# Regrouping seven products and twelve output triples in the second MLP of an attention-MLP kernel

## What is computed

```python
h = x @ w_in;  x = (h - tanh(h)) @ w_out                         # first MLP
h = x @ w_in;  sp = log1p(exp(h))                                # second MLP (sp = h above 20)
out = (h * tanh(sp)) @ w_out
```

## Time and profile before

| | us |
|---|---|
| median of 3 runs | 827.98 |
| lowest, highest | 826.56, 829.07 |
| profiled execution | 828.11 |
| its span | 826.3 |
| TensorE matmuls busy in it | 809.6 |
| VectorE busy | 544.3 |
| ScalarE busy | 363.7 |
| GpSimd busy | 149.8 |

### The profile page before, as it was taken

How to read it: one execution, slowest core, us unless ns; L and a number is a source line. 1 busy time by engine, 2 the same in 40 slices (tenths; PEclk the granted TensorE clock), 3 DMA queues, 4 the chain that set the end, 5 groups by cost and what they waited for, 6 DMA issues and landing times.

```text
span 826.3 us, 13419 instructions
## 1 busy us (share of the span) xinstructions
PE 809.6 (98%) x5340; PEld 761.8 (92%) x5340; DVE 544.3 (66%) x821; ACT 363.7 (44%) x571; POOL 149.8 (18%) x212
## 2 busy tenths in 40 slices
PE   4999999999999999999999999999999999999998
PEld 3999999999999999999999888888988888988896
DVE  5766555555556555534446788888877777877775
ACT  4544434433343434334335455546435445535434
POOL 3230344424404423410110021110000000000000
PEclk9999999999999999999999999999999999999999
DMA  7553345425434534422655255488424266523302
GB/s 249 169 173 112 103 160 202 164 101 192 167 115 167 179 119 160 180 65 90 230 175 182 90 194 202 151 326 309 180 90 159 109 253 240 207 90 120 148 1 77
DMA packets 41597, 132.21 MB, mean 160 GB/s; under 512 B 7104, under 2 KB 10944, under 8 KB 41536
## 3 DMA queue, kind: packets, MB, share of 16 engines
q1 hardware_dynamic: 29088, 83.38, 28.3%
q0 software_dynamic: 12448, 47.98, 16.5%
HBM read 91.49 MB, written 35.91 MB: 154 GB/s over the span
## 4 chain that ended last, share of the span: by engine, by line
PE 89%; DVE 6%; ACT 2%; DMA 1%; issue 1%; SPq 1%; DVEq 0%; ACTq 0%
PE psum L909 8%; PE psum L911 8%; PE psum L910 8%; PE psum L896 7%; PE psum L898 7%; PE psum L897 7%; PE psum L1030 7%; PE psum L1031 7%; PE psum L1029 7%; PE psum L1008 6%; PE psum L1009 6%; PE psum L1007 6%; PE psum L863 1%; PE psum L832 1%; DMA pool_words<-kT 1%
## 5 line engine op out<-in xcount | busy, mean ns | idle before, releaser
L651 DVE TENSOR_TENSOR pool_words<-psum,pool_words 128x384 f32<-128x384 f32 x96 | 53.4, 557 | 121.7 <-ACT pool_words L457 121.7
L909 PE MATMUL psum<-g_hi,w_hi 128*128 128x384 f32 x384 | 128.4, 334 | 0.6 <-DMA pool_words<-pool_words 0.6
L911 PE MATMUL psum<-g_hi,w_lo 128*128 128x384 f32 x384 | 128.3, 334 | 0.0
L910 PE MATMUL psum<-g_lo,w_hi 128*128 128x384 f32 x384 | 128.3, 334 | 0.0
L896 PE MATMUL psum<-x_hi,w_hi 128*128 128x384 f32 x360 | 122.2, 339 | 0.7 <-DVE w_lo L598 0.7
L897 PE MATMUL psum<-x_lo,w_hi 128*128 128x384 f32 x360 | 120.3, 334 | 0.0
L898 PE MATMUL psum<-x_hi,w_lo 128*128 128x384 f32 x360 | 120.3, 334 | 0.0
L457 ACT ACTIVATE pool_words<-psum 128x384 f32<-128x384 f32 x96 | 46.9, 489 | 147.8 <-PE psum L898 144.8
L1008 PE MATMUL psum<-w_lo,w_hi 128*128 128x384 f32 x288 | 97.5, 339 | 0.0
L1009 PE MATMUL psum<-w_hi,w_lo 128*128 128x384 f32 x288 | 97.0, 337 | 0.0
L1007 PE MATMUL psum<-w_hi 128*128 128x384 f32 x288 | 96.3, 334 | 0.0
(11 more groups left out here) (105 smaller groups left out, 1525.4 us busy)
## 6 DMA issues: line engine op xcount, KB each, us to landing
w_hi<-s_hi SPq DMA_DIRECT2D x24, 896.0 KB, 4.6
w_lo<-s_lo SPq DMA_DIRECT2D x24, 896.0 KB, 6.8
pool_words<-w_out POOLq DMA_DIRECT2D x32, 256.0 KB, 3.9
w_hi<-t_hi SPq DMA_DIRECT2D x18, 384.0 KB, 5.0
w_lo<-t_lo SPq DMA_DIRECT2D x18, 384.0 KB, 5.8
pool_words<-w POOLq DMA_DIRECT2D x24, 256.0 KB, 3.7
pool_words<-qT SPq DMA_DIRECT2D x18, 256.0 KB, 3.6
pool_words<-kT SPq DMA_DIRECT2D x18, 256.0 KB, 4.4
```

The costliest lines, as they stand in the source:

```text
L909: pe.matmul(ps, w_hi[:, 1, cols], g_hi[:, s, :], start=f == 0, stop=False)
L910: pe.matmul(ps, w_hi[:, 1, cols], g_lo[:, s, :], start=False, stop=False)
L911: mm = pe.matmul(ps, w_lo[:, 1, cols], g_hi[:, s, :], start=False, stop=f == FT - 1)
```

## The change

TRIPLES_AFTER goes from (2, 2, 1, 1, 1, 3, 2) to (0, 4, 0, 4, 0, 4, 0). With the order M1, M6, M7, M4, M2, M5, M3 this gives, in pairs 2 to 23: M1 M6, four triples, M7 M4, four triples, M2 M5, four triples, M3, and at once M1 and M6 of the next pair. Twelve triples a pair, as before; none follows M3. The order in pairs 0 and 1 on TensorE stays, and the waits of all products and triples are the same in number and place.

The loops of ScalarE and VectorE are written anew for iterations 2 to 24, and iterations 0 and 1 are written out ahead of them. Iteration `pair` now begins with the square term of the upper unit and take_c12 of the pair before. The diff:

```diff
@@ -40,7 +40,7 @@
 
 TOKEN_STEPS = (M1, M5, M3, M7, M6, M2, M4)
 
-TRIPLES_AFTER = (2, 2, 1, 1, 1, 3, 2)
+TRIPLES_AFTER = (0, 4, 0, 4, 0, 4, 0)
 
 
 FIRST_SCORES_AT = 1
@@ -561,32 +561,38 @@
                 act.activation(out_sb[:, j, :], y2_ps[j], ACT.Copy).then_inc(out_kept_act, 1)
 
             act.preload_act_table_set("natural_log_exp_and_others")
-            for pair in range(ALL_PAIRS + 1):
+            keep_m1(0)
+            u_exp(0)
+            inverse(0)
+            u_exp(1)
+            unit_hi(0)
+            inverse(1)
+            keep_y(GROUPS - 1)
+            keep_m1(1)
+            unit_hi(1)
+            u_exp(2)
+            for pair in range(2, ALL_PAIRS + 1):
+                upper, lower = 2 * pair - 2, 2 * pair - 1
                 seam = pair // PAIRS - 1 if pair % PAIRS == 1 and pair > PAIRS else None
-                if pair > 0:
-                    u_exp(2 * pair - 1)
-                if 1 < pair < ALL_PAIRS or pair == 0:
+                inverse(upper)
+                if pair < ALL_PAIRS:
                     keep_m1(pair)
+                u_exp(lower)
+                unit_hi(upper)
                 if seam is not None:
                     keep_out(seam, 0)
-                if pair > 0:
-                    unit_hi(2 * pair - 2)
-                    inverse(2 * pair - 1)
-                if pair == 1:
-                    keep_y(GROUPS - 1)
-                    keep_m1(pair)
+                inverse(lower)
                 if seam is not None:
                     keep_out(seam, 2)
+                unit_hi(lower)
+                if seam is not None:
                     keep_out(seam, 4)
-                if pair > 0:
-                    unit_hi(2 * pair - 1)
                 if pair in LATE_STEP_AT:
                     step_hi(LATE_STEP_AT[pair])
                 if pair in LATE_SPLIT_AT:
                     split_w2_out_hi(LATE_SPLIT_AT[pair])
                 if pair < ALL_PAIRS:
                     u_exp(2 * pair)
-                    inverse(2 * pair)
             for j in range(0, OUT_TILES, 2):
                 keep_out(SUPERS - 1, j)
 
@@ -771,46 +777,55 @@
                     dve.wait_ge(out_stored[j], 16 * s)
                 dve.tensor_copy(out_sb[:, j, :], y2_ps[j]).then_inc(out_kept_dve, 1)
 
-            for pair in range(ALL_PAIRS + 1):
+            for take in (take_u2, take_u3, take_c21, take_c11, take_c22):
+                take(0)
+            clamp(0)
+            square_term(0)
+            take_c12(0)
+            clamp(1)
+            gate(0)
+            square_term(1)
+            unit_lo(0)
+            keep_y(GROUPS - 1)
+            gate(1)
+            take_u2(1)
+            take_u3(1)
+            take_c21(1)
+            unit_lo(1)
+            take_c11(1)
+            take_c22(1)
+            clamp(2)
+            for pair in range(2, ALL_PAIRS + 1):
+
+                upper, lower = 2 * pair - 2, 2 * pair - 1
                 seam = pair // PAIRS - 1 if pair % PAIRS == 1 and pair > PAIRS else None
-                if pair > 0:
-                    gate(2 * pair - 2)
-                    square_term(2 * pair - 1)
-                if 1 < pair < ALL_PAIRS or pair == 0:
+                square_term(upper)
+                take_c12(pair - 1)
+                clamp(lower)
+                gate(upper)
+                if pair < ALL_PAIRS:
                     take_u2(pair)
+                square_term(lower)
+                unit_lo(upper)
                 if seam is not None:
                     keep_out(seam, 1)
-                if pair > 0:
-                    unit_lo(2 * pair - 2)
-                if 1 < pair < ALL_PAIRS or pair == 0:
+                if pair < ALL_PAIRS:
                     take_u3(pair)
-                if pair == 1:
-                    keep_y(GROUPS - 1)
-                if pair > 0:
-                    gate(2 * pair - 1)
-                if pair == 1:
-                    take_u2(pair)
-                    take_u3(pair)
+                    take_c21(pair)
                 if seam is not None:
                     keep_out(seam, 3)
-                if pair < ALL_PAIRS:
-                    take_c21(pair)
-                if pair > 0:
-                    unit_lo(2 * pair - 1)
+                gate(lower)
+                unit_lo(lower)
                 if seam is not None:
                     keep_out(seam, 5)
-                if pair < ALL_PAIRS:
-                    take_c11(pair)
                 if pair in LATE_STEP_AT:
                     step_lo(LATE_STEP_AT[pair])
                 if pair in LATE_SPLIT_AT:
                     split_w2_out_lo(LATE_SPLIT_AT[pair])
                 if pair < ALL_PAIRS:
+                    take_c11(pair)
                     take_c22(pair)
                     clamp(2 * pair)
-                    square_term(2 * pair)
-                    take_c12(pair)
-                    clamp(2 * pair + 1)
             for j in range(1, OUT_TILES, 2):
                 keep_out(SUPERS - 1, j)
 
```

## The result

Over 22 runs each, the changed kernel takes 829.76 us (median; 827.66 to 830.88) and the kernel before 827.07 us. The ratio is 1.003 with a 95% interval of 1.0023 to 1.0037, so the change costs 1.9 to 3.1 us. The forecast was 829.6 us.

A forecast was written before the change was run, and what follows sets the result against it. The prediction took TensorE, busy 809.6 of 826.3 us, as the bound. Matmul density -2.65, new waits +3.25, seam copies +0.15 and the end +0.85 sum to +1.6 us on 827.98: forecast 829.6 us, range 827.0 to 832.3.

The forecast's parts named there:

- density: TensorE, 22 pairs: fewer changes between 384- and 512-column matmuls save 0.12 us a pair, -2.65 us in all.
- waits of pairs 3 to 8: M6 waits for take_c12 behind VectorE's token steps and splits: 4.05 us, less 0.78 of present waits, +3.25 us.
- seams: Two pairs behind a seam: three copies join the queue, two of them behind take_c21, +0.15 us for both.
- end: After pair 23's last M3, only twelve triples cover the chain to unit 47: +0.85 us, from +0.7 to +1.4.
- the product behind four triples: TensorE: the product following a run of four triples pays extra, between 0 and 0.03 us, taken as 0.015.
- The ring: Cycle from one take_c12 to the next through TensorE and VectorE: 15.95 us in iterations 3 and 6, against TensorE's 15.61.
- The 0.60 for the sum: Iterations 2, 4 and 5: GpSimd's token add makes the clamp end 0.60 us later, raising the stall to 0.94.
- M3's waits: Product M3 waiting for take_c22 in pairs 2 to 8 of the kernel before: 0.78 us, which would go.
- Rival A: M6 misses take_c12 in every pair, by 0.15 us in 15 pairs: +2.25, 831.9 us; chance 0.15.
- Rival B: The matmul density gain does not come, because change of width is not the cost: 832.2 us; chance 0.08.
- rival C: VectorE's queue is looser than added up, pairs 3 to 8 stall no more than now: 826.4 us; chance 0.12.
- D: The change only trades one wait for another and pairs keep 15.73 us: 828.0 us; chance 0.05.

The follow-up runs named there:

- runs-of-two kernels: Kernel before with tuple (2, 2, 2, 0, 2, 2, 2): alone 827.08 us; with step_lo and split behind clamp(upper) and old tuple in pair 23, 825.0 us.
- The short sums: Changed kernel with the third super's GpSimd token sums over 8 columns instead of 384; one run, M1(2) to M1(9) 111.08 us.
- the early step_lo: Changed kernel with step_lo ahead of take_u3, the split behind clamp(upper) and step_hi moved forward on ScalarE; 825.6 us, ratio 0.9977 to the kernel before.
- the first experiment: Changed kernel with step_lo and the split moved behind clamp(upper) on VectorE; 830.41 us, ratio 1.0034 to the kernel before.
- the grouping alone: Kernel before with only TRIPLES_AFTER changed to (0, 4, 0, 4, 0, 4, 0), old VectorE and ScalarE queues; 829.15 us, ratio 1.0017.

## Why the prediction was right

Each term of the forecast that has bounds lies within them.

| term | forecast | measured |
|---|---|---|
| density, 22 pairs | -2.65 (-3.5 to -1.2) | -1.91 |
| waits of pairs 3 to 8, less those of before | +3.25 | +3.2 |
| seams | +0.15 | +0.12 |
| end | +0.85 | +0.75 |
| sum | +1.6 | +2.2 |

- **Density.** The step that was mis-sized is the product behind four triples, "I take 0.015, the middle". It pays about 0.026, near the upper bound of 0.03, as behind three triples: 3 x 0.067 us in a pair instead of 3 x 0.055. That makes 22 x 0.087 us. The idea that fewer changes of width bring the gain was incomplete: the runs-of-two kernels have twice as many runs and the same pace. By the starts in the timelines, less the dense pace, a run with the product behind it costs 0.040 us for one triple, 0.033 for two, 0.066 for three and 0.067 for four. What makes a run of two so cheap was not looked into.
- **The ring.** Forecast 0.34 for iterations 3 and 6, 0.94 for 2, 4 and 5 and 0.55 for 7; measured 0.33, 0.93 and 0.55. The short sums show the same ring without GpSimd, and the early step_lo takes both parts away. The 0.60 for the sum was right in size because its rows had the order that the changed kernel has: the split ahead of the sum, the clamp behind it. The reading that a split "that starts inside the add is not blocked" was wrong; the first experiment failed on it. The ring as summed is that of the new queues: with the old ones, in "the grouping alone", the same total falls on other pairs.
- **M3's waits** are gone from pairs 3, 5 and 6, as forecast.
- **The end.** M1(23) to the last triple is 0.66 us longer, and without pair 23's own density gain of 0.09 it is the 0.75 of the table. The waits are 1.01 us ahead of unit 46 and 0.39 ahead of unit 47, each with 0.1 for the slow second matmul. The chain from M3 is 0.6 us shorter, where 0.5 was taken.
- **Rival A** did not happen, but by 0.05 us, less than the 0.1 that the forecast put. Rival B is ruled out by the quiet pairs and rival C by pairs 3 to 8. D's exchange of one wait for another is real, yet the quiet pairs are faster.
- **The base.** The forecast counted from 827.98, the median of the three runs shown; over 22 runs it is 827.07. So its +1.6 us stands against a measured +2.5 (1.9 to 3.1) and lies below the interval, by the density term above all (0.74 us). That 829.6 is so near the measured 829.76 is luck: a base 0.9 us too high and a change 0.9 us too small cancel. The traces show +2.2, so some 0.3 us of the runs' difference has no place in the sum.

## What to carry to other kernels

Where the bound engine's stream is dense, add up the ring through the queue that feeds it before regrouping. Here a product that reuses a bank one product later had a slack of about 0.05 us, and side work in that queue then landed on the bound engine. The gain could be had without that price, by runs of two, which keep four triples between a bank's reader and its next writer; but in the runs' times it showed only together with the moved steps and the old tuple in pair 23. Before moving side work that sets off GpSimd, look at what VectorE does next: here it cost nothing where VectorE next read PSUM.

## What the runs showed of the hardware

- A GpSimd add and a VectorE instruction with both inputs in SBUF run one after the other, whichever starts first, but for the last 0.15 us or so. Held behind the add, a square term took 2.59 us and a multiply 1.41 (0.96 alone), both ending 0.81 us behind it; a clamp with one input (0.56 alone) is held too and ended 0.42 behind it. Behind a split the add took 2.2 us, behind a square term 2.63, alone 1.85. The takes, with one input from PSUM, kept their 0.55 us beside it.
- The pace of matmuls of two widths depends on how they are grouped, by 0.033 (two triples) to 0.067 us (four) a run, and not simply on the number of changes.
- When take_c12 ended 0.16 us ahead of M6's first matmul, the second still came 0.24 us behind the first instead of 0.17; when it ended 0.29 ahead, it did not.
